# Round and copy order of a fused attention, MoE and mixture kernel: weight copies held back beside the routing arithmetic, the index wait moved into later rounds, the mixture's last two row blocks one after the other

## The reference, cut to what matters

```python
# attention: B=2, H=8, S=768, D=64; keys kept: the first n_global=8 and the n_local=96 latest
a = softmax(scale * q @ k.T - slope[h] * dist, over kept keys)
x = (a @ v) laid out as [1536, 512]
# first mixture (MoE): each row goes to ONE of 8 experts
expert_idx = argmax(normalised(x) @ normalised(expert_emb).T / tau)
gate_w = softmax(logits)[expert_idx]
x = gate_w * (relu(x @ w1[expert_idx]) @ w2[expert_idx])     # 512 -> 1024 -> 512
# second mixture: each row goes through ALL of 4 experts
p = domain_probs / sum(domain_probs)
out = sum over e of p[:, e] * (relu(x @ moe2_w1[e]) @ moe2_w2[e])
```

## Time and profile before

| what | us |
|---|---|
| median of 3 runs (904.0 to 907.66) | 907.46 |
| the profiled execution, its own time | 905.01 |
| its span in the profile | 903.2 |
| TensorE busy | 844.7 |
| VectorE, ScalarE, GpSimd busy | 287.8, 261.8, 291.1 |
| mean granted TensorE clock | 0.981 |

### The profile page before, as it was taken

One profiled execution on the slowest core, in us unless ns is written; L12 is line 12 of the kernel. 1 busy time (PEld: TensorE's weight loads), 2 busy tenths in 40 slices (PEclk: granted clock), 3 DMA queues, 4 the chain that ended last, 5 costly groups with the idle time before them and its releaser, 6 DMA issues.

```text
span 903.2 us, 13860 instructions
## 1 busy us (share of the span) xinstructions
PE 844.7 (94%) x4913; PEld 710.0 (79%) x4913; DVE 287.8 (32%) x797; ACT 261.8 (29%) x578; POOL 291.1 (32%) x161
## 2 busy tenths in 40 slices
PE   8999969766999999999999999999999999999996
PEld 5666659766999999878787878787878787878784
DVE  6877758851222231121212121212121212121211
ACT  5888855332545454111111111111111111111110
POOL 1520018573888887100164000164000065010101
PEclk9999979897999999999999999999999999999999
DMA  5776524326666666100033000033000000010101
GB/s 171 264 233 227 196 85 142 116 25 228 193 193 195 192 187 185 47 1 1 0 93 93 1 0 0 0 90 97 1 0 0 0 0 0 1 46 0 46 0 47
DMA packets 28024, 76.68 MB, mean 85 GB/s; under 512 B 6600, under 2 KB 6984, under 8 KB 27984
## 3 DMA queue, kind: packets, MB, share of 16 engines
q1 hardware_dynamic: 25584, 68.30, 24.5%
q0 software_dynamic: 2400, 7.87, 2.9%
HBM read 69.85 MB, written 6.30 MB: 84 GB/s over the span
## 4 chain that ended last, share of the span: by engine, by line
PE 86%; DVE 6%; DMA 2%; ACT 2%; issue 2%; SPq 1%; DVEq 0%; POOL 0%; ACTq 0%
PE ps L1368 29%; PE ps L1361 29%; PE ps L1325 9%; PE ps L1311 8%; PE ps L1205 3%; PE ps L1231 3%; PE ps L1217 3%; PE ps L1153 1%; DMA token_of<-tokd 1%; PE ps L1245 1%; DVE parts L1002 1%; DVE h L1121 1%; ACT h L634 1%; DMA win<-qkv 1%; PE ps L1300 1%
## 5 line engine op out<-in xcount | busy, mean ns | idle before, releaser
L1368 PE MATMUL ps<-ring,h 128*128 128x512 f32 x1152 | 276.4, 390 | 17.9 <-DVE h L1121 17.9
L1361 PE MATMUL ps<-x2T,ring 128*128 (+1 forms) x1152 | 275.0, 389 | 0.0
L1368 PEld LDWEIGHTS ps<-ring,h 128*128 128x128 f32 x1152 | 215.3, 188 | 67.4 <-DVE h L1121 23.0
L1361 PEld LDWEIGHTS ps<-x2T,ring 128*128 128x128 f32 x1152 | 216.1, 188 | 44.8
L279 POOL TENSOR_TENSOR ring<-raw,ring 128x1024 fp32r<-128x1024 f32 x96 | 230.4, 2408 | 61.0 <-ACT ring L587 57.5
L634 ACT ACTIVATE h<-ps 128x512 fp32r<-128x512 f32 x96 | 57.5, 599 | 476.6 <-PE ps L1361 476.6
L1121 DVE SCALAR_TENSOR_TENSOR h<-ps,h 128x512 fp32r<-128x512 f32 x96 | 66.4, 692 | 396.8 <-ACT h L634 396.8
L1325 PE MATMUL ps<-hT,ring 128*128 128x256 f32 x768 | 107.5, 291 | 21.2 <-DVE hT L1067 19.8
L500 POOL CAST ring<-raw 128x1024 fp32r<-128x1024 f32 x24 | 25.0, 1042 | 312.8 <-PE ps L1361 266.4
L1325 PEld LDWEIGHTS ps<-hT,ring 128*128 128x128 f32 x768 | 99.1, 196 | 23.7 <-DVE hT L1067 20.8
L1311 PE MATMUL ps<-x1T,ring 128*128 (+1 forms) x768 | 104.3, 286 | 1.7 <-DVE x1T L1062 1.7
(11 more groups left out here) (155 smaller groups left out, 424.2 us busy)
## 6 DMA issues: line engine op xcount, KB each, us to landing
raw<-wts SPq DMA_DIRECT2D x96, 512.0 KB, 3.9
win<-qkv SPq DMA_DIRECT2D x32, 320.0 KB, 3.1
win<-qkv SPq DMA_DIRECT2D x8, 384.0 KB, 4.5
x_rows<-xrow SPq DMA_DIRECT2D x12, 256.0 KB, 3.2
xrow<-consts SPq DMA_DIRECT2D x1, 768.0 KB, 4.5
xg<-x_rows,idx_now POOLq DMA_INDIRECT x14, 4.3
result<-acc,tokd POOLq DMA_INDIRECT x12, 2.7
idx_all<-token_of SPq DMA_DIRECT2D x10, 0.5 KB, 2.0
```

The source lines that it names most:

```text
L1361: ins = nc.tensor.matmul(ps[:, 4 + f % 2, :], w1(wp, f, k), x2T[:, xp * KD + k, bass.ds(g * 512, 512)], start=(k == 0 and n == 0), stop=(k ...
L1368: ins = nc.tensor.matmul(ps[:, t, :], h2[:, f % 2, hp_, t * P:t * P + P], w2(wp, f, 0, DM), start=(f == 0 and n == 0), stop=(f == KF - 1 a ...
```

## The change

1. `group` of the second mixture projects all row blocks in order: block 6 whole, then block 7 whole, each with its own wait. y2_ready rises in block 7, three matmuls apart.
2. GpSimd copies and splits all eight quarters of the first unit during attention. SyncE loads all eight quarters of the second unit there too.
3. ScalarE copies no weights in chunk -1 until f = 5: then q0, two after f = 6, two after f = 7; in chunk 0 two after f = 1, q7 after f = 2, and from there as before. `gate_exps` is at f = 4.
4. VectorE's tables are packed differently: `gate_logits` at f = 3 with `token_homes`, `gates` at 5, `gate_parts` at 6 of chunk -1 with the second half of `spot`, `pack(0)` at 7; in chunk 0 `pack(1)` at 1, `number_extras` at 2, `choose_extras` at 3, `read_order` at 5, `read_extras` at 6. The copy of `origin` into `parts` moves into attention.
5. `find_order` on TensorE moves from f = 5 to f = 3 of chunk 0.
6. VectorE waits for idx_more once, between rounds 4 and 5 of its loop, which is cut in two for it.
7. `keep_busy` ahead of the first chunk has 16 matmuls in place of 32.

```diff
@@ -41,7 +41,6 @@
 QW = F
 XW = B * S + CH
 ROUNDS = S // P
-FILLED = 6
 
 
 def fused_kernel(nc, qkv, limits, emb, tau, probs, wts, consts, out):
@@ -376,7 +375,7 @@
             def beside_attention(m):
 
                 u, j = divmod(m // 2, NQ)
-                if m % 2 == 0 and m and m // 2 < NQ + FILLED:
+                if m % 2 == 0 and m and m // 2 < 2 * NQ:
                     if u:
                         sp.wait_ge(split_done, j + 1)
                     load_quarter(sp, u, j, raw_ready)
@@ -410,10 +409,9 @@
                 sp.dma_start(raw[:, j, :], wts[bass.ds(u, 1), :, j * QW:j * QW + QW].rearrange(
                     "u p c -> (u p) c")).then_inc(raw_ready[j], 16)
 
-            for c in range(1, 3):
-                for j in range(FILLED if c == 1 else 0, NQ):
-                    sp.wait_ge(split_done, NQ * (c - 1) + j + 1)
-                    load_quarter(sp, c, j, raw_ready)
+            for j in range(NQ):
+                sp.wait_ge(split_done, NQ + j + 1)
+                load_quarter(sp, 2, j, raw_ready)
             sp.wait_ge(order_found, 1)
             sp.dma_start(tok_dram.rearrange("(t p) -> p t", p=P), tokd[:, :], allow_slow_non_contiguous=True).then_inc(tok_stored, 16)
             sp.wait_ge(tables_ready, 1)
@@ -441,7 +439,7 @@
         @block.gpsimd
         def _(pool):
             nc.gpsimd.memset(order_b[:, :, :], 0.0).then_inc(idle_ready, 1)
-            for j in range(FILLED):
+            for j in range(NQ):
                 pool.wait_ge(raw_ready[j], 16)
                 nc.gpsimd.tensor_copy(ring[:, j, 0, :], raw[:, j, :]).then_inc(high_pool, 1)
                 pool.wait_ge(high_pool, j + 1)
@@ -453,10 +451,10 @@
                         out=xg[:, h, :], out_offset=None, in_=x_dram,
                         in_offset=bass.IndirectOffsetOnAxis(ap=idx[:, h:h + 1], axis=0)).then_inc(gathered[h], 16)
 
-            def lows(c, first, end):
+            def lows(p, first, end):
 
                 for j in range(first, end):
-                    pool.wait_ge(high_act, c * NQ + (j - FILLED + 1))
+                    pool.wait_ge(high_act, p * NQ + (j + 1))
                     low_part(j, split_done)
 
             pool.wait_ge(x_stored, 16 * NT)
@@ -464,26 +462,23 @@
             gather(idx_all[:, 0:2])
             pool.wait_ge(xT_psum, 2)
             gather(idx_all[:, 2:4])
-            lows(0, FILLED, NQ)
-            lows(1, 0, 4)
+            lows(0, 0, 4)
             pool.wait_ge(idx_next, 1)
-            lows(1, 4, 5)
+            lows(0, 4, 5)
             gather(idx_now)
-            lows(1, 5, FILLED)
+            lows(0, 5, NQ)
             pool.wait_ge(count_ready, 1)
             prev = pool.value_load(last_i[0:1, :], min_val=E - 2, max_val=CHUNKS - 2)
             last = prev + 1
-            with pool.Fori(1, last) as c:
-                lows(c, FILLED, NQ)
-                lows(c + 1, 0, 4)
-
-                pool.wait_ge(idx_next, c + 1)
-                lows(c + 1, 4, 5)
+            with pool.Fori(1, last) as p:
+                lows(p, 0, 4)
+
+                pool.wait_ge(idx_next, p + 1)
+                lows(p, 4, 5)
                 gather(idx_now)
-                lows(c + 1, 5, FILLED)
+                lows(p, 5, NQ)
             for h in range(2):
                 pool.wait_ge(gathered[h], last * 16 + 32)
-            lows(last, FILLED, NQ)
 
             for j in range(NQ):
                 pool.wait_ge(high2_act, j + 1)
@@ -586,18 +581,14 @@
                         act.wait_ge(projected, p * KF + (j + 1))
                 nc.scalar.copy(ring[:, j, 0, :], raw[:, j, :]).then_inc(high2_act if second else high_act, 1)
 
-            def chunk(p, final=False, beside=None):
+            usual = [(), ((0, 6),), ((0, 7),), ((1, 0),), ((1, 1),), ((1, 2),), ((1, 3),), ((1, 4), (1, 5))]
+
+            def chunk(p, turns=usual, final=False, beside=None):
 
                 for f in range(1, KF):
                     relu_high(p, f)
-                    if f == 1:
-                        high_part(p, 6, False)
-                    elif f == 2:
-                        high_part(p, 7, False)
-                    else:
-                        high_part(p + 1, f - 3, final)
-                    if f == 7:
-                        high_part(p + 1, 5, final)
+                    for after, j in turns[f]:
+                        high_part(p + after, j, final and after)
                     if not final and f in (4, 5):
                         x_high_part(p + 1, f - 4)
                     if beside and f == beside[0]:
@@ -610,11 +601,11 @@
             x_high_part(-1, 0)
             x_high_part(-1, 1)
             relu_high(-1, 0)
-            chunk(-1, beside=(5, gate_exps))
+            chunk(-1, [(), (), (), (), (), ((1, 0),), ((1, 1), (1, 2)), ((1, 3), (1, 4))], beside=(4, gate_exps))
             relu_high(0, 0)
             act.wait_ge(off_ready, 1)
             y_high_part(0)
-            chunk(0)
+            chunk(0, [(), ((0, 5), (0, 6))] + usual[2:])
             act.wait_ge(tables_ready, 1)
             prev = act.value_load(last_i[0:1, :], min_val=E - 2, max_val=CHUNKS - 2)
             last = prev + 1
@@ -711,6 +702,7 @@
 
                 dve.wait_ge(route_ready, 16 * 2)
                 nc.vector.memset(onehot[:, NT, :], 0.0)
+                nc.vector.tensor_copy(parts[:, :, 0:2], origin)
                 step(nc.vector.tensor_reduce(dsum[:, :, 0], dprob[:, :, :], AX.X, ALU.add))
                 step(nc.vector.tensor_scalar(dsum[:, :, 0], dsum[:, :, 0], 1e-9, None, ALU.add))
                 step(nc.vector.reciprocal(dsum[:, :, 0], dsum[:, :, 0]))
@@ -999,7 +991,6 @@
 
             def gate_parts():
 
-                route(nc.vector.tensor_copy(parts[:, :, 0:2], origin))
                 route(nc.vector.tensor_copy(parts[:, :, 2:6], dprob[:, :, :]))
                 route(nc.vector.tensor_tensor(rest[:, 0], dprob[:, :, :], parts[:, :, 2:6], ALU.subtract))
                 route(nc.vector.tensor_copy(parts[:, :, 6:10], rest[:, 0]))
@@ -1097,20 +1088,24 @@
             x_low_part(-1, 0)
             x_low_part(-1, 1)
             hidden_part(-1, 0)
-            chunk(-1, beside={1: [token_rounds], 2: [token_offsets], 3: [token_homes],
-                             4: [gate_logits], 5: [lambda: spot(lanes, 0, homes_ready, [0])], 6: [gates],
-                             7: [lambda: spot(lanes, 0, homes_ready, [1])]})
+            chunk(-1, beside={1: [token_rounds], 2: [token_offsets], 3: [token_homes, gate_logits],
+                              4: [lambda: spot(lanes, 0, homes_ready, [0])], 5: [gates],
+                              6: [gate_parts, lambda: spot(lanes, 0, homes_ready, [1])], 7: [lambda: pack(0)]})
             hidden_part(0, 0)
             y_low_part(0)
-            chunk(0, beside={1: [gate_parts], 2: [lambda: pack(0)], 3: [lambda: pack(1)], 4: [number_extras],
-                             5: [choose_extras], 6: [read_order, read_extras], 7: [write_tables]})
+            chunk(0, beside={1: [lambda: pack(1)], 2: [number_extras], 3: [choose_extras], 5: [read_order],
+                             6: [read_extras], 7: [write_tables]})
             dve.wait_ge(count_ready, 1)
             prev = dve.value_load(last_i[0:1, :], min_val=E - 2, max_val=CHUNKS - 2)
             last = prev + 1
-            with dve.Fori(1, prev) as p:
+            with dve.Fori(1, E - 3) as p:
                 hidden_part(p, 0)
                 y_low_part(p)
-                dve.wait_ge(idx_more, 16 * 2 * (CHUNKS - E))
+                chunk(p)
+            dve.wait_ge(idx_more, 16 * 2 * (CHUNKS - E))
+            with dve.Fori(E - 3, prev) as p:
+                hidden_part(p, 0)
+                y_low_part(p)
                 chunk(p)
             hidden_part(prev, 0)
             y_low_part(prev)
@@ -1376,29 +1371,25 @@
                     if f % 2 == 0:
                         pe.wait_ge(split2_done, NQ * e + f + 2)
 
-                for f in range(KF - 2):
-                    hidden2(e, g, f + 1)
+                for f in range(KF):
+                    if f + 1 < KF:
+                        hidden2(e, g, f + 1)
                     may_project(f)
                     if f == 0 and banks_free:
                         banks_free()
                     for t in range(4):
                         ins = project2(e, g, f, t)
-                    ins.then_inc(hid_used, 1)
-                hidden2(e, g, KF - 1)
-                may_project(KF - 2)
-                may_project(KF - 1)
-                for t in range(4):
-                    ins = project2(e, g, KF - 2, t)
-                    if t == 3:
+                        if f == KF - 1:
+                            ins.then_inc(y2_ready, 1)
+                    if f < KF - 1:
                         ins.then_inc(hid_used, 1)
-                    project2(e, g, KF - 1, t).then_inc(y2_ready, 1)
-
-            keep_busy(32)
+
+            keep_busy(16)
             turn_x(-1, 0)
```

(2 more changed lines are left out.)

## The result

The changed kernel takes **876.85 us** (median of 4 runs, 874.97 to 877.38); beside it the kernel before took 906.98. The ratio is 0.967, with a 95% interval of 0.9654 to 0.9687. The profiled execution took 877.03, of which 875.2 are span (before: 905.01 and 903.2): 28.0 us less, where the forecast had 18.2.

What follows compares the result with a forecast made beforehand. TensorE, busy 844.7 of 903.2 us, was taken to bound the kernel, its waits next. The terms summed as 905.0 - 19.6 - 1.0 + 0.5 + 1.9 = 886.8, forecast 887 us, range 866 to 893.

Steps and rivals of the forecast that it cites:

- Second mixture, -19.6: Second mixture: in-order blocks remove 12 waits and speed the 24 matmuls behind, -21.2 us; later last stores +1.6.
- Fewer keep-busy matmuls, -1.0: Ahead of the first chunk: 16 matmuls instead of 32 let rows be turned earlier; -1.0 us, bounds -1.6 and +0.1.
- Two more quarters in attention, +0.5: Attention: q7's subtraction on GpSimd meets a bias scaling on VectorE; +0.5 us, from 0 to 1.2.
- First mixture, +1.9: First mixture: dense subtractions delay VectorE, order found at 195.0, chunk 2's first project at 236.2 against 234.3; +1.9 us.
- where no gap stands between two of them, VectorE did not get in: First mixture: back-to-back GpSimd subtractions hold a VectorE instruction to the run's end; TensorE loses 7.6 and 6.0 us.
- three signs that the prediction gave for being wrong: First mixture: small instructions ending between back-to-back subtractions, order found before 185, or reload not following it by 21 us.
- The chain through SyncE: First mixture: 21.0 us from order found to first reload, quarter landing 3.9 later, then ScalarE's copy; 7 us wait in chunk 1.
- gains 193.2 less the time of the order: First mixture: formula for this stage's gain in us, from the time at which the order is found.
- One subtraction at a time: First mixture: GpSimd's next subtraction lets a waiting VectorE instruction in first; order at 188, total 880 us; chance 0.17.
- Collision in chunk -1 alone: First mixture: VectorE's small instructions collide with subtractions only in chunk -1; order at 185, total 877 us; chance 0.12.
- the mechanism that the forecast rested on: First mixture: subtraction runs hold VectorE to their end in chunks -1 and 0; 887 to 890 us; chance 0.50.

Runs made afterwards that it cites:

- e3: Kernel before with only the second mixture's row blocks projected in order: 885.84 us, ratio 0.977.
- e8: Changed kernel with keep_busy put back from 16 to 32 matmuls: 879.50 us, ratio 0.9696.
- e2: Kernel before with only the copy of origin moved from gate_parts into attention: 906.84 us, one run.
- e4: Kernel before with only VectorE's wait for the further indices moved behind round 4: 901.83 us, ratio 0.9948.
- e9: Kernel before with one more tensor_reduce, its result unused, ahead of the copy of origin in gate_parts: 908.38 us, one run.
- e6: Changed kernel with gates and gate_parts moved ahead of GpSimd's first run of four subtractions: 880.25 us, ratio 0.9698.
- e7: Changed kernel with unit 3 loaded ahead of the order, and gates and gate_parts ahead of GpSimd's first run: 872.32 us, ratio 0.9616.
- e10: e7 with number_extras moved ahead of chunk -1's first hidden part and choose_extras into its block 1: 866.92 us, ratio 0.9562.

## Why the forecast was right, and where it was not

- **Second mixture, -19.6.** Measured -20.08 from the start of the stage. The wait, the full stream of 24 matmuls and the end of the program (3.05 us, forecast 3.0) came as worked out. Alone (e3) it is -20.08 in the trace too, with the same end.
- **Fewer keep-busy matmuls, -1.0.** The first hidden came 0.47 us earlier than before although attention ended 0.90 later: -1.37. The clock did not fall ahead of it; it was at half only from 122.14 to 128.97. What 16 of these matmuls cost hangs on the clock: put back into the changed kernel they cost 2.50 us (e8).
- **Two more quarters in attention, +0.5.** The scaling met the subtraction as said: 1.85 us at 59.56 where it had taken 0.43. Attention is 0.90 longer, of which some 0.4 were there before that place. One pair of traces can't settle this size: the first gather stands at 121.38 to 123.13 in the five runs built on the kernel before, and at 121.63 to 123.61 in the seven built on the changed one.
- **First mixture, +1.9. This is the step that failed:** measured -7.45, which is most of the 9.8 us by which the sum missed. The sentence was "where no gap stands between two of them, VectorE did not get in". It was read from the 9.50 us row and taken for the rule of every dense run, though the same trace had the run at 136.41 with an instruction let in between two of its subtractions. The runs show two kinds. A run that follows a gather at once holds VectorE to its end (9.50, 9.51, 9.22, 12.24, 12.25, 7.06 us); a run that begins out of a wait lets one in at each boundary. The change made dense runs, but of the second kind. For chunk -1 both readings give nearly the same, since five instructions and four boundaries fill the run: 6.70 us against 7.6 forecast. In chunk 0 `number_extras` cost TensorE nothing and `choose_extras` 1.40 us, instead of 6.0 for the first, and the clock was not lost there. Two of the three signs that the prediction gave for being wrong came: small instructions ended between two back-to-back subtractions, and the order was found before 185 (184.92).
- **The chain through SyncE.** Right in size: 21.2 us from the order to the first reload (forecast 21.0), landed 3.8 later, ScalarE's copy then, and TensorE behind it. The formula "gains 193.2 less the time of the order" holds: the first mixture starts 0.47 us earlier than before, so 184.92 is 185.4 on the axis of before, the gain 7.8, against 7.45 measured.
- **The rivals.** "One subtraction at a time" had the true mechanism for these runs, with the order at 188; it came at 185.4 on the axis of before, because chunk 0's first project came 1.1 us earlier than forecast (167.08, which is 167.6 on that axis, against 168.7), block 3 was not late at all (three of the six instructions of `number_extras` are reduces, which took 0.49, 0.20 and 0.18 inside the run) and block 4 was 1.4 late, not 2.3. "Collision in chunk -1 alone", order at 185, 877, had the true time, without the reason: small instructions did meet the subtractions of chunk 0, at a low price. Together they had 0.29. That the time lies within the range is owed to the range taking both in, and not to the mechanism that the forecast rested on, which had 0.50. That the forecast's direction was never in doubt rests on the second mixture, which was right.
- **The rule of the ports.** In the changed kernel the waits end at the subtraction's end. The Trainium skill (SBUF — State Buffer, "Who interferes with whom") says the first to issue has the shared pair for its whole instruction; these rows agree, 2.08 to 2.33 us against subtractions of 2.34. It says nothing of a hold across several; the 9.50 us row, where the prediction set trace against rule, is real and comes back in e2, e3, e4, e9, e6, e7 and e10, but only behind a gather; in the first mixture of all 14 traces no run that began out of a wait held an instruction over 3.4 us. The same page of the Trainium skill ("SBUF: two separate sides") says that GpSimd needs the pair to write a gather's descriptors; the rows are divided on it. For it: L939, which was held from 0.37 us inside a gather, and the gather of 1.77 us at 162.29 in e6, beside `pack`. Against it: in the changed kernel `pack` began 0.10 us inside a gather, and both took their usual time:

```profile
161.98 0.94 POOL L450 DMA_INDIRECT xg<-x_rows,idx_now  x1 [0.30 <-issue]
```

```profile
162.08 1.20 DVE L1002 TENSOR_TENSOR packs<-homes,parts 128x1008 bf16<-128x1008 bf16 x1
```

Why the hold goes on through the run no page of the Trainium skill says and no run shows: it was not tried with another instruction than a gather ahead of the run, nor with a pause that is not a wait for the gather's landing.
